# MoE with block transposes into PSUM, sorted rows in two buffers and loads three tiles ahead

## What is computed

```python
logits = x @ w_gate
e_idx = np.argmax(logits, axis=1)
...
for e in range(E):                      # 8 experts
    mask = e_idx == e
    h = np.maximum(x[mask] @ w1[e], 0.0)    # 512 -> 1024
    ye = h @ w2[e]                          # 1024 -> 512
    out[mask] = gate_w[mask, None] * eom[mask, e, None] * ye
...
h = x @ w_in                            # 512 -> 2048
g = h - np.tanh(h)
return (g @ w_out).astype(np.float32)
```

## Time and profile before

| what | value |
|---|---|
| median of three executions | 1078.49 us |
| the profiled execution, its device time | 1082.62 us |
| its span in the profile | 1080.8 us (1.8 us of the time lie around it) |
| TensorE matmuls busy | 1022.5 us, 95% of the span |
| TensorE weight loads busy | 844.5 us, 78% |
| VectorE busy | 722.2 us, 67% |
| ScalarE busy | 305.9 us, 28% |
| GpSimd busy | 389.5 us, 36% |
| mean granted TensorE clock | 0.985 of full speed |
| MoE stage, first matmul of hidden(0) to the last copy of rows | 143.85 to 514.9 us |

### The profile page before, as it was taken

One profiled execution on the slowest core, in us unless ns is written; L12 is line 12 of the kernel. 1 busy time (PEld: TensorE's weight loads), 2 busy tenths in 40 slices (PEclk: granted clock), 3 DMA queues, 4 the chain that ended last, 5 costly groups with the idle time before them and its releaser, 6 DMA issues.

```text
span 1080.8 us, 18667 instructions
## 1 busy us (share of the span) xinstructions
PE 1022.5 (95%) x5744; PEld 844.5 (78%) x5745; DVE 722.2 (67%) x1246; ACT 305.9 (28%) x540; POOL 389.5 (36%) x325
## 2 busy tenths in 40 slices
PE   7888868999999999999889999999999999999998
PEld 6777757878887778777778887887887888788887
DVE  3666674645555566555388768877777886887775
ACT  1111112223222222231123333333333333333333
POOL 4478668577595975935700000000000000000000
PEclk9999988999999999999899999999999999999999
DMA  9899747676776776764200010001001001000101
GB/s 334 285 318 316 256 147 224 226 259 220 228 245 221 250 242 221 249 216 167 84 10 13 18 40 19 19 0 49 19 10 49 19 10 39 19 0 0 39 1 39
DMA packets 70969, 138.37 MB, mean 128 GB/s; under 512 B 7056, under 2 KB 39184, under 8 KB 70928
## 3 DMA queue, kind: packets, MB, share of 16 engines
q1 hardware_dynamic: 21888, 73.41, 20.5%
q10 hardware_dynamic: 45200, 51.82, 14.9%
q0 software_dynamic: 3840, 12.59, 3.6%
HBM read 98.73 MB, written 39.06 MB: 127 GB/s over the span
## 4 chain that ended last, share of the span: by engine, by line
PE 77%; DVE 8%; DMA 8%; issue 3%; ACTq 2%; ACT 1%; POOL 0%; DVEq 0%; POOLq 0%
PE banks L1122 15%; PE banks L1124 15%; PE banks L1123 15%; PE banks L1214 8%; PE banks L1215 8%; PE banks L1216 8%; DMA hid_rows<-hid 3%; PE banks L1061 3%; DMA xs_sb<-x_sorted 2%; PE banks L1007 2%; PE banks L1050 2%; DVE probs L724 2%; DMA ident<-in_small 1%; PE banks L1193 1%; DVE hidT L864 1%
## 5 line engine op out<-in xcount | busy, mean ns | idle before, releaser
L383 POOL TENSOR_TENSOR w_sb<-raw,w_sb 128x1024 fp32r<-128x1024 f32 x80 | 198.0, 2475 | 6.7
L396 POOL DMA_INDIRECT gathered<-y_sorted,row_back x20 | 22.1, 1104 | 374.7 <-DVE x_sb L924 374.1
L1214 PE MATMUL banks<-x2T_hi,w_sb 128*128 (+1 forms) x384 | 153.0, 398 | 4.2 <-DVE g_sb L959 4.2
L1216 PE MATMUL banks<-x2T_lo,w_sb 128*128 (+1 forms) x384 | 150.7, 393 | 0.0
L1215 PE MATMUL banks<-x2T_hi,w_sb 128*128 (+1 forms) x384 | 150.7, 392 | 0.0
L1124 PE MATMUL banks<-w_sb,g_hi 128*128 128x512 f32 x384 | 149.4, 389 | 0.0
L1122 PE MATMUL banks<-w_sb,g_lo 128*128 128x512 f32 x384 | 149.4, 389 | 0.0
L1123 PE MATMUL banks<-w_sb,g_hi 128*128 128x512 f32 x384 | 149.4, 389 | 0.0
L1122 PE MATMUL banks<-w_sb,xsT_lo 128*128 (+1 forms) x248 | 100.2, 404 | 21.5 <-DVE xsT_lo L823 21.5
L630 ACT ACTIVATE square<-banks 128x512 f32<-128x512 f32 x96 | 57.4, 598 | 195.9 <-PE banks L1216 195.9
L637 ACT ACTIVATE g_hi<-g_sb 128x512 fp32r<-128x512 f32 x96 | 60.7, 632 | 163.3 <-PE banks L1124 146.6
(11 more groups left out here) (128 smaller groups left out, 1786.7 us busy)
## 6 DMA issues: line engine op xcount, KB each, us to landing
raw<-in_weights SPq DMA_DIRECT2D x80, 512.0 KB, 4.4
in_sb<-in_rows SPq DMA_DIRECT2D x48, 512.0 KB, 6.2
hid_rows<-hid ACTq DMA_DIRECT2D x31, 512.0 KB, 3.3
hid_quads<-hid_rows ACTq DMA_DIRECT2D x31, 512.0 KB, 3.9
xs_sb<-x_sorted ACTq DMA_DIRECT2D x124, 64.0 KB, 3.4
y_sorted<-ys_sb ACTq DMA_DIRECT2D x31, 256.0 KB, 3.7
out_rows<-out_sb SPq DMA_DIRECT2D x24, 256.0 KB, 2.1
x_sorted<-zeros ACTq DMA_DIRECT2D x1, 2048.0 KB, 21.6
```

What stands on the lines that cost most here:

```text
L383: nc.gpsimd.tensor_tensor(w_sb[:, s, 1, lo:hi], raw[:, p % RAW_SLOTS], w_sb[:, s, 0, lo:hi].bitcast(fp32), ALU.subtract).then_inc(piece_do ...
L1214: T.matmul(out_, w_lo, hi, start=first, stop=False)
L1216: return T.matmul(out_, w_hi, lo, start=False, stop=last)
```

## The change

It has five parts.

1. `xsT` and `hidT` are no longer tensors in SBUF but PSUM banks: 0 for `xsT`, 3 and 6 for the halves of `hidT`. VectorE's block transposes write there, the copies of ScalarE and the subtractions of VectorE read there. Warm-up matmuls that wrote to bank 0 now write to bank 1.
2. `xs_sb`, `xsT_hi` and `xsT_lo` exist twice, and a tile's rows are loaded three tiles ahead instead of two.
3. VectorE's step i is now: copy_rows(i-3), transpose_rows(i+1), x_lo(i+1), transpose_hidden(i-1), hid_lo(i-1). Before, transpose_hidden(i-1) stood ahead of x_lo(i+1).
4. ScalarE's step i is now: store_rows(i-3), x_hi(i+1), relu(i), store_hidden(i), load_rows(i+3), hid_hi(i-1), load_hidden(i). Before, it was relu(i) with store_rows(i-3) between its halves, store_hidden(i), x_hi(i+1), hid_hi(i-1), load_hidden(i), load_rows(i+2).
5. The chain of gates and rows on VectorE is cut into four pieces that stand behind steps 0, 1, 2 and 3, and the two exponentials on ScalarE stand behind step 0. GpSimd no longer waits for x_lo(0) before it splits the second expert's weights.

```diff
@@ tiles
-    xs_sb = c_.place("xs_sb", [P, QUADS, D // QUADS])
-    xsT = c_.place("xsT", [P, DK, P])
-    xsT_hi = c_.place("xsT_hi", [P, DK, P], fp32r)
-    xsT_lo = c_.place("xsT_lo", [P, DK, P], fp32r)
+    xs_sb = c_.place("xs_sb", [P, 2, QUADS, D // QUADS])
+    xsT_hi = c_.place("xsT_hi", [P, 2, DK, P], fp32r)
+    xsT_lo = c_.place("xsT_lo", [P, 2, DK, P], fp32r)
...
-    hidT = c_.place("hidT", [P, FK, P])
...
+        xsT = at(0)
+        hidT = [at(3), at(6)]
@@ gpsimd
-            pool.wait_ge(xsT_lo_done, 1)
             pool.wait_ge(tables_done, 1)
             split_pieces(0, 1)
@@ scalar
             def moe_step(i, number):
 
-                relu(i, 0)
                 if number >= 3:
                     store_rows(i - 3)
+                if number + 1 < MOE_TILES:
+                    x_hi(i + 1, number + 1)
+                relu(i, 0)
                 relu(i, 1)
                 store_hidden(i, number)
-                if number + 1 < MOE_TILES:
-                    x_hi(i + 1)
+                if number + 3 < MOE_TILES:
+                    load_rows(i + 3, number + 3)
                 if number >= 1:
                     hid_hi(i - 1, number - 1)
                 load_hidden(i)
-                if number + 2 < MOE_TILES:
-                    load_rows(i + 2)
@@ vector
                 if number + 1 < MOE_TILES:
-                    transpose_rows(i + 1)
+                    transpose_rows(i + 1, (number + 1) % 2)
+                    x_lo(i + 1, (number + 1) % 2)
                 if number >= 1:
                     transpose_hidden(i - 1)
-                if number + 1 < MOE_TILES:
-                    x_lo(i + 1)
-                if number >= 1:
                     hid_lo(i - 1, (number - 1) % 2)
 
-            for i in range(5):
-                moe_step(i, i)
+            moe_step(0, 0)
+            gate_scores()
+            moe_step(1, 1)
+            token_scales()
+            moe_step(2, 2)
+            rows_before()
+            moe_step(3, 3)
+            rows_after()
+            moe_step(4, 4)
@@ vector, how hidT's halves are written
-                    V.transpose(hidT[:, ks].rearrange("p k (b g) -> p g k b", g=QUADS),
+                    V.transpose(hidT[n].rearrange("p (k b g) -> p g k b", k=DK, g=QUADS),
                                 hid_quads[:].rearrange("p g (k a) -> p g k a", k=FK)[:, :, ks]).then_inc(hidT_done, 1)
```

More of the change, by code:

```diff
@@ L249, in build_program @@
         piece_done = sem("piece_done")
-        xs_ready = sem("xs_ready")
+        xs_ready = [sem(f"xs_ready{n}") for n in range(2)]
         xsT_done = sem("xsT_done")
@@ L596, in _ @@
                 act.wait_ge(x_scattered[n], 16 * (TOKEN_TILES // X_RING))
-            load_rows(0, first=True)
-            x_hi(0)
+            load_rows(0, 0)
+            x_hi(0, 0)
             act.wait_ge(tables_done, 1)
-            load_rows(1)
+            load_rows(1, 1)
+            load_rows(2, 2)
+            moe_step(0, 0)
             act.wait_ge(shifted_done, 1)
@@ L821, in x_lo @@
-            def x_lo(i):
+                V.transpose(xsT.rearrange("p (k g b) -> p g k b", k=DK, g=QUADS),
+                            xs_sb[:, par].rearrange("p g (k a) -> p g k a", k=DK)).then_inc(xsT_done, 1)
+            def x_lo(i, par):
                 dve.wait_ge(xsT_hi_done, i + 1)
-                V.tensor_tensor(xsT_lo[:].rearrange("p a n -> p (a n)"), xsT[:].rearrange("p a n -> p (a n)"),
-                                xsT_hi[:].rearrange("p a n -> p (a n)").bitcast(fp32), ALU.subtract).then_inc(xsT_lo_done, 1)
@@ L852, in _ @@
-            link(V.tensor_scalar(tile_row[:], row_at[:], ROW_BITS - (P - 1), None, ALU.bitwise_and))
-            link(V.tensor_tensor(per_tile[1][:], tile_row[:], per_tile[1][:], ALU.subtract))
-            V.scalar_tensor_tensor(out=row_back[:], in0=per_tile[1][:], scalar=0.0, in1=per_tile[0][:],
-                                   op0=ALU.max, op1=ALU.add).then_inc(rows_back_done, 1)
+                V.tensor_tensor(xsT_lo[:, par].rearrange("p a n -> p (a n)"), xsT,
+                                xsT_hi[:, par].rearrange("p a n -> p (a n)").bitcast(fp32), ALU.subtract).then_inc(xsT_lo_done, 1)
@@ new lines, in _, with gate_scores, token_scales @@
+            transpose_rows(0, 0, first=True)
+            x_lo(0, 0)
+            over_tokens = [P, TOKEN_TILES, EXPERTS]
+            def gate_scores():
+                link(V.tensor_tensor(gate_all[:], output_gate, onehot[:], ALU.mult))
+                link(V.reduce_sum(per_tile[0][:], gate_all[:], AX))
+                V.tensor_tensor(shifted[:], router, over_experts(top[:]), ALU.subtract).then_inc(shifted_done, 1)
+            def token_scales():
+                dve.wait_ge(exp_done, 2)
+                link(V.reduce_sum(top[:], shifted[:], AX))
+                link(V.tensor_scalar(top[:], top[:], 1e-9, None, ALU.add))
+                link(V.tensor_scalar(per_tile[1][:], per_tile[1][:], 1.0, None, ALU.add))
+                link(V.reciprocal(top[:], top[:]))
+                link(V.reciprocal(per_tile[1][:], per_tile[1][:]))
+                link(V.tensor_tensor(token_scale[:], top[:], per_tile[1][:], ALU.mult))
@@ new lines, in rows_before @@
+            def rows_before():
+                first_tile, move = per_expert[0], per_expert[7]
+                link(V.tensor_tensor(first_tile[:], through[:], tiles[:], ALU.subtract))
+                link(V.scalar_tensor_tensor(out=move[:], in0=first_tile[:], scalar=float(P), in1=region_row,
+                                            op0=ALU.mult, op1=ALU.subtract))
+                link(V.tensor_tensor(gate_all[:], move[:].unsqueeze(1).to_broadcast(over_tokens), onehot[:], ALU.mult))
+                link(V.reduce_sum(per_tile[0][:], gate_all[:], AX))
+                link(V.tensor_tensor(per_tile[0][:], per_tile[0][:], row_at[:], ALU.add))
@@ new lines, in rows_after @@
+            def rows_after():
+                link(V.tensor_tensor(gate_all[:], last_start[:].unsqueeze(1).to_broadcast(over_tokens), onehot[:], ALU.mult))
+                link(V.reduce_sum(per_tile[1][:], gate_all[:], AX))
+                link(V.tensor_scalar(tile_row[:], row_at[:], ROW_BITS - (P - 1), None, ALU.bitwise_and))
+                link(V.tensor_tensor(per_tile[1][:], tile_row[:], per_tile[1][:], ALU.subtract))
+                V.scalar_tensor_tensor(out=row_back[:], in0=per_tile[1][:], scalar=0.0, in1=per_tile[0][:],
+                                       op0=ALU.max, op1=ALU.add).then_inc(rows_back_done, 1)
@@ L1124, in split_product, with hidden @@
                 return T.matmul(out_, hi, w_lo, start=False, stop=last)
-            def hidden(i, first=False):
+            def hidden(i, par, first=False):
                 if first:
@@ L1160, in rows_out @@
                 last.then_inc(ys_done, 1)
-            stay_warm(WARM_TAIL[2], still, 0)
-            stay_warm(WARM_TAIL[3], still, 0)
-            hidden(0, first=True)
+            stay_warm(WARM_TAIL[2], still, 1)
+            stay_warm(WARM_TAIL[3], still, 1)
+            hidden(0, 0, first=True)
             pe.wait_ge(tables_done, 1)
-            hidden(1)
+            hidden(1, 1)
             def moe_step(i, number):
-                hidden(i)
+                hidden(i, number % 2)
                 rows_out(i - 2, number, number % 2)
@@ L1178, in _ @@
                 if i < MOE_TILES:
-                    hidden(i)
+                    hidden(i, i % 2)
                 rows_out(i - 2, i, i % 2)
```

57 lines of the change are left out of this document (19 added, 38 removed).

## The result

The changed kernel takes 1068.7 us as the median of 4 runs (1068.19 to 1069.74), against 1078.41 before. The ratio is 0.9916 (95% interval 0.9901 to 0.9931): faster, by 9.7 us, just under half of the 19.5 that were forecast. A second measurement with a fresh set of runs gave 1066.1 us and 0.9883 (0.9857 to 0.9910), 12.4 us. All 69 runs of the kernel before that were made over the study lie between 1073.4 and 1084.6 us.

What follows compares the result with a forecast made beforehand. TensorE, 95% busy, was taken as the bound, so only its idle or slow-clock time could go. Gains of 11.9 (loop), 7.1 (start) and 0.5 (end) sum to 19.5 us: median 1078.5 to 1059, range 1053 to 1069.

Steps and rivals of the forecast that it cites:

- Gain at the start 7.1 us: MoE stage up to hidden(5): 17.7 us of excess become 9.1 lost plus 1.5 for the slow clock.
- Steps 1 and 2: Starts of hidden(1) and hidden(2), each waiting for relu of the tile before: 1.2 us lost at each.
- Step 3: rows_out(0) waits for hid_lo(0), since ScalarE passes store_hidden(1) and load_rows(4) before hid_hi(0): 0.9 us lost.
- Step 4: hidden(3) starts late behind token_scales, x_lo(3) and relu(2,1): 0.15 us lost.
- Step 5: rows_out(1) waits for copy_rows(0), which stands behind rows_before on VectorE: 4.3 us lost, a new wait.
- The clock: Slow clock at the start, behind the gap of 4.3 us: an estimated 1.5 us lost.
- Step 6: rows_out(2) waits for copy_rows(1), behind hid_lo(2) and 3.75 us of rows_after: 1.4 us lost.
- the start eats its gain: Rival: slow landings, GpSimd holding rows_before and a second slow stretch leave 0 to 3 of 7.1: about 1065; chance 0.18.
- loop and end: MoE from hidden(5) on: all nine loop waits go, 11.9 us gained, and the end gains 0.5.
- The rival of slow strided transposes: VectorE's transposes into PSUM take 2.2 us a half instead of 1.08; loop holds, time 1065; chance 0.09.
- Waits for relu: Sign of a wrong prediction if in the loop; rival of no change, 1075 to 1081, chance 0.06.
- The coupling of ScalarE and VectorE: Rival of a slower kernel: late landings of hid hold up relu each step, 1084 or 1109; chance 0.05.

Runs made afterwards that it cites:

- before_again: The kernel before, profiled once more with no edit: 1078.8 us, ratio 1.0004.
- loads_two: The changed kernel with rows loaded two tiles ahead instead of three: 1067.7 us, ratio 0.9894 against the kernel before.
- loads_early: The kernel before with load_rows(i+2) ahead of hid_hi(i-1) and load_hidden(i) on ScalarE, all tiles in SBUF and single: 1071.2 us, ratio 0.9927.
- psum_only: The kernel before with part 1 alone, xsT and hidT in PSUM: 1069.8 us, ratio 0.9900.
- order_only: The kernel before with x_lo(i+1) ahead of transpose_hidden(i-1) on VectorE: 1085.6 us, ratio 1.0059.
- in_sbuf: The changed kernel with xsT and hidT as SBUF tensors again: 1072.6 us, ratio 0.9942 against the kernel before.
- psum_hidden: The kernel before with hidT alone in PSUM, xsT in SBUF: 1073.9 us, ratio 0.9934.
- psum_rows: The kernel before with xsT alone in PSUM, hidT in SBUF: 1074.6 us, ratio 0.9946.

## Why the prediction came out as it did

The direction held, and 1068.7 still lies in the range 1053 to 1069, at its very edge; the size did not. 19.5 us were forecast, 9.7 and 12.4 measured. Two steps of the sum failed: the gain at the start, and the loop's waits of one profile, which stood above the median, counted in full as a gain of the median.

**The step that failed: "Gain at the start 7.1 us".** Between the first profiles the start's excess went from 17.7 to 14.3, and from 17.7 to 13.3 between the second ones: 3.4 and 4.4. Steps 1 and 2 were right (0.88 and 1.11 us of wait, with breaks 1.2 and 1.4). Step 3 had 0.9 and it was 1.82 of wait, 2.1 with the break: load_hidden(0) landed 15.1 us behind the start of hidden(0) instead of 14.1, and the issue of the four loads behind it took 2.45 us instead of 1.8. Step 4 had 0.15 and lost 0.4. Step 5 had 4.3 and it was 5.92 of wait, 6.2 with the break, because rows_before was costed at 3.75 us from its old place; in the new one more of its short instructions met GpSimd. The clock had 1.5 and 13 slow matmuls cost 13 x 0.2 = 2.6. Step 6's 1.4 did not occur, since rows_out(1) itself was late and rows_after took 1.4 us instead of 3.75. The rival "the start eats its gain" names two of these causes, GpSimd and the clock, and its 1065 lies nearer the result.

**The reference of the sum: "it stood 4.1 above the median, so the median goes from 1078.5 to 1059".** The prediction took 4.1 us off both sides, as if the profiled execution's surplus over the median were constant. In before_again, which stands 0.4 us above its median, it is gone, and with it 4.7 us of the loop, so the surplus was part of the gain counted. Between the first profiles rest fell by 13.2 us, between the second ones by 8.5, against 12.4 forecast for loop and end. With 3.4 to 4.4 at the start this gives 16.6 and 12.9 for the MoE. The second agrees with the second pair of medians, 12.4. Why the first measurement showed only 9.7 stays open; the intervals of the two ratios meet only at 0.990 to 0.991. A candidate that the prediction did not have lies outside the MoE: the changed kernel's first profile began it 2.3 us later than that of before, the second one 0.9 us earlier. A late start of 2 to 3 us in the first four runs would make 12.9 about 10; no run shows whether they had it.

**The loop: right result, wrong account of the cause.** All nine waits went, as said. But the prediction laid this to loads three ahead and the second buffers, and gave PSUM 0.5 us. The runs show otherwise: the distance is worth nothing (loads_two), the buffers are not needed (loads_early and psum_only have single ones), and what held the loads was their place in the order of ScalarE's queue. Moving load_rows ahead of hid_hi and load_hidden frees the loop in SBUF (loads_early). PSUM alone frees it too, which is shown, but not how: it shortens transpose_hidden, behind which hid_hi and the next loads stand, and it also shortens the way from the rows' landing to x_lo, and no run separates the two. In order_only, where hid_hi comes later, the loop's waits are 9.2 us and the start's excess is 3.1 us larger. The parts do not add up: psum_only wins about 9 to 10, the rest without PSUM (in_sbuf) 5 to 6, both together 10 to 12. The mechanism by which psum_hidden and psum_rows each give half is open.

**PSUM.** The bound that I chose, 1.08 us for transposes with stride, was wrong by a third: 0.70, below even the lower bound of 0.71. The rival of slow strided transposes is refuted: the stride has a price in SBUF (1.08 against 0.71 us) and none in PSUM (0.70 against 0.72). Of 93 subtractions with one SBUF input none lasted over 0.693 us, where with two the longest was 2.88.

The Trainium skill ("SBUF — State Buffer", Door 1: The DMA port swizzle, its note on cachelines) gives PSUM lines of 8 bytes and says that access there that is not contiguous slows matmuls; it gives no figure for VectorE. For this transpose the trace shows no price. The Trainium skill ("SBUF — State Buffer", Who interferes with whom) says that a VectorE instruction with two SBUF inputs contends with a GpSimd instruction that reads SBUF, and that one with at most one does not, outside the modes that use two ports. The subtractions agree. But an instruction of the chain with one SBUF input was long too, and ended at 169.19 us, where a weight split of 2.38 us on GpSimd ended at 169.16; no run tells in which mode it ran, so one input alone is no safe sign:

```profile
167.13 2.06 DVE L848 TENSOR_SCALAR top<-top 128x24 f32<-128x24 f32 x1
169.22 0.18 DVE L849 TENSOR_SCALAR per_tile<-per_tile 128x24 f32<-128x24 f32 x1
```

**The other rivals.** Waits for relu came at the start only (0.88, 1.11). The coupling of ScalarE and VectorE that would make it slower did not occur in the changed kernel, but order_only is a relative of it.
